# Second MoE of an FFT and two-MoE kernel: seven Strassen products in place of eight block products

## What is computed

```python
def reference(x, moe_w_in, moe_w_out, moe2_w_in, moe2_w_out, moe2_alpha):
    X = np.fft.fft(np.fft.fft(x, axis=1), axis=2).real     # x: 2 x 3008 x 256
    X = X.reshape(6016, 256)
    h = X @ moe_w_in                                        # 256 x 2048
    X1 = (h / (1 + np.exp(-h))) @ moe_w_out                 # 2048 x 256
    h = X1 @ moe2_w_in
    g = np.maximum(h, 0) + moe2_alpha * np.minimum(h, 0)
    return g @ moe2_w_out                                   # 6016 x 256
```

## Time and profile before

| | |
|---|---|
| median of 3 runs | 970.4 us (970.27 to 970.58) |
| profiled execution | 971.95 us |
| its span, first to last instruction | 970.1 us |
| PE matmul, busy | 960.3 us, 99%, 4186 matmuls |
| PE weight loads, busy | 785.5 us, 81% |
| DVE, busy | 433.7 us, 45% |
| ACT, busy | 575.3 us, 59% |
| POOL, busy | 495.7 us, 51% |
| granted TensorE clock | 1.0 (2.4 GHz) throughout |

### The profile page before, as it was taken

One profiled execution on the slowest core, in us unless ns is written; L12 is line 12 of the kernel. 1 busy time (PEld: TensorE's weight loads), 2 busy tenths in 40 slices (PEclk: granted clock), 3 DMA queues, 4 the chain that ended last, 5 costly groups with the idle time before them and its releaser, 6 DMA issues.

```text
span 970.1 us, 10736 instructions
## 1 busy us (share of the span) xinstructions
PE 960.3 (99%) x4186; PEld 785.5 (81%) x4186; DVE 433.7 (45%) x627; ACT 575.3 (59%) x681; POOL 495.7 (51%) x240
## 2 busy tenths in 40 slices
PE   9999999999999999999999999999999999999998
PEld 4578887888888888878888888888888888888887
DVE  6779974655544544554443232322223233232321
ACT  2475654676666666667665556555555655655554
POOL 0197553477656555565755444444535354444533
PEclk9999999999999999999999999999999999999999
DMA  9512000011000000000000000000000000000000
GB/s 347 210 55 64 1 1 1 22 33 54 23 1 22 1 1 0 1 1 23 22 22 1 22 0 22 1 22 22 1 21 1 22 1 22 22 1 21 1 22 22
DMA packets 12776, 27.94 MB, mean 29 GB/s; under 512 B 1290, under 2 KB 8500, under 8 KB 11700
## 3 DMA queue, kind: packets, MB, share of 16 engines
q1 hardware_dynamic: 12628, 27.21, 7.9%
q0 software_dynamic: 96, 0.03, 0.0%
HBM read 21.03 MB, written 6.21 MB: 28 GB/s over the span
## 4 chain that ended last, share of the span: by engine, by line
PE 89%; DVE 5%; POOL 2%; ACT 1%; issue 1%; DMA 1%; SPq 0%; ACTq 0%; DVEq 0%; POOLq 0%
PE ps L309 12%; PE ps L311 12%; PE ps L310 12%; PE ps L561 9%; PE ps L566 9%; PE ps L560 9%; PE ps L526 7%; PE ps L522 7%; PE ps L523 7%; POOL gl L1047 2%; PE ps L470 2%; PE ps L422 1%; DVE h_sb L971 1%; PE ps L454 1%; DVE x_tile L793 1%
## 5 line engine op out<-in xcount | busy, mean ns | idle before, releaser
L1047 POOL TENSOR_TENSOR gl<-g_sb,gh 128x1004 fp32r<-128x1004 f32 x192 | 419.6, 2186 | 430.0 <-ACT gh L700 267.7
L1007 DVE SCALAR_TENSOR_TENSOR g_sb<-h_sb,neg_alpha,g_sb 128x502 f32<-128x502 f32 x192 | 160.4, 877 | 349.9 <-ACT g_sb L695 349.9
L700 ACT CAST gh<-g_sb 128x1004 fp32r<-128x1004 f32 x96 | 99.1, 1032 | 137.9 <-DVE g_sb L1007 137.9
L522 PE MATMUL ps<-gh,wo 128*128 128x502 f32 x384 | 148.0, 386 | 1.0 <-DVE x L961 0.8
L561 PE MATMUL ps<-gh,wo 128*128 128x502 f32 x384 | 148.6, 387 | 0.0
L523 PE MATMUL ps<-gh,wo 128*128 128x502 f32 x384 | 148.4, 386 | 0.0
L309 PE MATMUL ps<-xs,wi 128*128 128x502 f32 x384 | 148.0, 385 | 0.0
L310 PE MATMUL ps<-xs,wi 128*128 128x502 f32 x384 | 148.0, 385 | 0.0
L311 PE MATMUL ps<-xs,wi 128*128 128x502 f32 x384 | 148.0, 385 | 0.0
L560 PE MATMUL ps<-gh,wo 128*128 128x502 f32 x384 | 147.3, 384 | 0.0
L971 DVE SCALAR_TENSOR_TENSOR h_sb<-n_all,a,v_sb 128x502 f32<-128x502 f32 x96 | 81.5, 849 | 144.9 <-ACT v_sb L732 144.9
(11 more groups left out here) (88 smaller groups left out, 1137.2 us busy)
## 6 DMA issues: line engine op xcount, KB each, us to landing
x_tile<-x_tiles SPq DMA_DIRECT2D x6, 1024.0 KB, 13.7
out_t<-out_sb SPq DMA_DIRECT2D x11, 502.0 KB, 2.8
stage<-moe_w_out SPq DMA_DIRECT2D x16, 256.0 KB, 2.8
n_parts<-n_rows SPq DMA_DIRECT2D x5, 502.0 KB, 3.8
w_sb<-moe_w_in SPq DMA_DIRECT2D x4, 512.0 KB, 8.6
stage<-moe_w_in SPq DMA_DIRECT2D x8, 256.0 KB, 4.2
t_sb<-t SPq DMA_DIRECT2D x1, 1134.0 KB, 17.8
t_sb<-t SPq DMA_DIRECT2D x3, 376.0 KB, 13.7
```

Source lines behind the costliest of these rows:

```text
L522: pe.matmul(dst, wh, gh[g % 2][:, sg, :], start=f == 0, stop=False)
L1007: ins = dve.scalar_tensor_tensor(out=gs[:, i, :], in0=m[:, i, :], scalar=neg_alpha[:, f:f + 1], in1=gs[:, i, :], op0=ALU.mult, op1=ALU.add)
L1047: pool.tensor_tensor(gl[g % 2][:, :, :], g_sb[g % 2][:, :, :], gh[g % 2][:, :, :].bitcast(F32), ALU.subtract).then_inc(gl_done, 1)
```

## The change

The product h = w_in^T x of the second MoE is taken as a 2 x 2 block product: w_in's inner features in two halves of 1024 (8 blocks of 128 each), its input features in two halves of 128, and the chunk's tokens in two halves of 502. Strassen's scheme makes the four blocks of h from seven products of sums of blocks. So for each of 48 units (6 chunks by 8 blocks, `UNITS`) there are 7 times `three` = 21 matmuls in place of 24, each product in a bank of its own (banks 0 to 3, three of them used twice). DVE forms the four 128x502 tiles of h from PSUM by seven additions (`half_sum`) into h4 in SBUF, the first of them with product 1, which ACT copies out of PSUM before (`copy_p1`). ReLU, PReLU, rounding and low part are then made from h4 in three portions, tile 0, tile 1, and tiles 2 and 3 together; before, ReLU read PSUM. The second product keeps its 24 matmuls per unit, tile by tile, in banks 4 to 7, all four of which are accumulated through a chunk, and its first half lies between products 7 and 2 of the next unit, its second half behind product 4.

The sums of blocks have to be made and split as well. Of w_in: 4 sums (POOL), 7 roundings (ACT) and 7 low parts (POOL), each in two portions of 512 columns, in steps 38 to 48 and 54 to 64 of the first MoE. Of x1: each chunk is stored to DRAM when it is done (SP) and four of its quarters are loaded back, then 4 sums, 7 low parts (POOL) and 7 roundings (ACT) of 502 columns per chunk, for chunk 0 in steps 71 to 89, for the others in units 1 to 6 of the chunk before. The xs operand and its split go. The eight stage splits of wo2 stand two before unit 0 and two each in units 1 to 3. When a chunk's second product is complete, in the lists of unit 8n of the next chunk, ACT copies banks 6 and 7 and DVE banks 4 and 5 into one output buffer, before PE may start the next chunk's sums in them.

The diff, cut to its core:

```diff
+PRODUCTS = {1: ("a11", "b11"), 6: ("s2", "t2"), 5: ("s1", "t1"), 7: ("s3", "t3"),
+            2: ("a12", "b21"), 3: ("s4", "b22"), 4: ("a22", "t4")}
+W_SETS = ["a11", "a12", "a22", "s1", "s3", "s2", "s4"]
+X_ROWS = ["b11", "b21", "b22", "t1", "t3", "t2", "t4"]
+TILES = [(1, 1), (0, 0), (0, 1), (1, 0)]
...
+        W_AT = [W2_AT + 8192 * i for i in range(4)] + [XS_AT, PQ_AT, PQ_AT + 8192]
...
+        W_SUMS = {"s1": ("a21", "a22"), "s3": ("a11", "a21"), "s2": ("s1", "a11"), "s4": ("a12", "s2")}
...
+        X_SUMS = {"t3": ("b22", "t1"), "t1": ("t1", "b11"), "t2": ("b22", "t1"), "t4": ("b21", "t2")}
+        X_HI = ["b11", "t1", "t4", "b21", "b22", "t3", "t2"]
+        X_STEP_SUM, X_STEP_HI, X_STEP_LO = 71, [75, 76, 77, 85, 86, 87, 88], [76, 77, 78, 86, 87, 88, 89]
...
+            def store_x1(c):
+                for i in range(2):
+                    sp.wait_ge(x1_done[i], c + 1)
+                sp.dma_start(x1_rows[c].rearrange("p a t -> p a t"),
+                             x1[:, c, :, :, :].rearrange("p s j t -> p (s j) t")).then_inc(x1_out, 16)
+            def load_xr(n):
+                sp.wait_ge(x1_out, 16 * max(n + 1, 4 if n == 0 else 0))
+                for k, x in enumerate(("b11", "b21", "t1", "b22")):
+                    sp.dma_start(xr_raw[n % 2][x][:, :], x1_rows[n, :, k, :]).then_inc(xr_in, 16)
...
+            sp.wait_ge(stage_hi, WO2_ITEM)
+            sp.wait_ge(stage_lo, WO2_ITEM)
+            load_w7(0)
+            store_x1(0)
             sp.wait_ge(t1_lo, len(T1_JOBS))
             sp.wait_ge(t23_lo, len(T23_JOBS))
             store_n(NC1 // 2, NC1)
             sp.wait_ge(n_out, 64)
             load_n(3)
-            for i in range(WI2_ITEM + 4, WO2_ITEM):
+            store_x1(1)
+            load_n(4)
+            store_x1(2)
+            sp.wait_ge(w7_lo, len(W_SETS))
+            load_w7(1)
+            load_n(5)
+            store_x1(3)
+            load_xr(0)
+            sp.wait_ge(w7_lo, 2 * len(W_SETS))
+            for i in range(WO2_ITEM, WO2_ITEM + SLOTS):
                 load_item(i)
-            load_n(4)
-            for i in range(WO2_ITEM, WO2_ITEM + 4):
+            store_x1(4)
+            store_x1(5)
+            sp.wait_ge(mm2, STEPS1)
+            load_xr(1)
+            for i in range(WO2_ITEM + SLOTS, len(items)):
                 load_item(i)
...
+            for n in range(NC1):
+                if 1 <= n < NC1 - 1:
+                    sp.wait_ge(prod_b, 3 * HF * n)
+                    load_xr(n + 1)
...
+            def product(u, p):
+                n, fp = divmod(u, HF)
+                w, x = PRODUCTS[p]
+                bank = {1: 0, 6: 1, 5: 2, 7: 3, 2: 0, 3: 1, 4: 2}[p]
+                wh, wl = (w7[w][:, i, fp * P:(fp + 1) * P] for i in range(2))
+                xh, xl = (xr[n % 2][x, i][:, :] for i in range(2))
+                return three(pe, ps[:, bank, 0:N], wh, wl, xh, xl, True, True)
+            def products_a(u):
+                n, fp = divmod(u, HF)
+                if u == 0:
+                    pe.wait_ge(h_done, STEPS1)
+                    pe.wait_ge(w7_lo, 2 * len(W_SETS))
                 if fp == 0:
...
+                    pe.wait_ge(xr_lo, len(X_ROWS) * (n + 1))
+                for i, p in enumerate((1, 6, 5, 7)):
+                    if u and i < 3:
+                        pe.wait_ge(comb, 7 * u - 2 + i)
+                    product(u, p).then_inc(prod_a, 1)
+            def products_b(u):
+                pe.wait_ge(p1_done, u + 1)
+                product(u, 2).then_inc(prod_b, 1)
+                pe.wait_ge(comb, 7 * u + 1)
+                product(u, 3).then_inc(prod_b, 1)
+                pe.wait_ge(comb, 7 * u + 2)
+                product(u, 4).then_inc(prod_b, 1)
+            def second2(u, k):
+                n, fp = divmod(u, HF)
+                half, sg = TILES[k]
+                f = fp + HF * half
                 if n == 0:
...
+                    pe.wait_ge(stage_lo, WO2_ITEM + 1 + WO2_ORDER.index(f // 2))
+                if fp == 0 and k < 2:
+                    pe.wait_ge(x1_done[sg] if n == 0 else out_done[sg], NC1 if n == 0 else n)
+                pe.wait_ge(gh_done, STEPS1 + 3 * u + min(k, 2) + 1)
+                out = [ps[:, 4 + 2 * sg + ft, 0:N] for ft in range(2)]
                 for ft in range(2):
...
+                    wh, wl = (wo2[:, f, i, ft * P:(ft + 1) * P] for i in range(2))
+                    pe.matmul(out[ft], wh, gh4[:, k, :], start=fp == 0 and k < 2, stop=False)
+                    pe.matmul(out[ft], wl, gh4[:, k, :], start=False, stop=False)
+                pe.wait_ge(gl_done, STEPS1 + 3 * u + min(k, 2) + 1)
+                for ft in range(2):
+                    ins = pe.matmul(out[ft], wo2[:, f, 0, ft * P:(ft + 1) * P], gl4[:, k, :],
+                                    start=False, stop=fp == HF - 1 and k >= 2)
...
+            for g in range(LAG, STEPS1):
+                first1(g)
+                second1(g - LAG)
                 if g in JOB_AFTER:
                     job(JOB_AFTER[g])
+            second1(STEPS1 - 2)
+            products_a(0)
+            second1(STEPS1 - 1)
+            products_b(0)
+            for u in range(1, UNITS):
+                products_a(u)
+                second2(u - 1, 0)
+                second2(u - 1, 1)
+                products_b(u)
+                second2(u - 1, 2)
+                second2(u - 1, 3)
+            for k in range(4):
+                second2(UNITS - 1, k)
...
+            def copy_p1(u):
+                act.wait_ge(prod_a, 4 * u + 1)
+                if u:
+                    act.wait_ge(comb, 7 * u - 2)
+                act.copy(p1_sb[:, :], ps[:, 0, 0:N]).then_inc(p1_done, 1)
+            def relu(u, k):
+                act.wait_ge(comb, 7 * u + (3, 5, 7)[k])
+                act.wait_ge(gl_done, STEPS1 + max(3 * (u - 1) + k + 1, 0))
+                ks = slice(k, k + 1 if k < 2 else 4)
+                act.activation(g4[:, ks, :], h4[:, ks, :], ACT.Relu)
+                act.activation(h4[:, ks, :], h4[:, ks, :], ACT.Relu, scale=-1.0).then_inc(relu_done, 1)
+            def split_g_hi(u, k):
+                act.wait_ge(g_done, 3 * u + k + 1)
+                act.wait_ge(mm2, STEPS1 + max(4 * (u - 1) + (k + 1 if k < 2 else 4), 0))
+                ks = slice(k, k + 1 if k < 2 else 4)
+                act.copy(gh4[:, ks, :], g4[:, ks, :]).then_inc(gh_done, 1)
...
+            split_hi(WO2_ITEM + 1)
+            for u in range(UNITS):
+                n, fp = divmod(u, HF)
+                copy_p1(u)
+                if u:
+                    split_g_hi(u - 1, 2)
+                if u == 0:
                     store_x1_minus(NC1 - 1)
-                if fp == LAG - 1 and n >= 1:
+                relu(u, 0)
+                if 1 <= u <= 3:
+                    split_hi(WO2_ITEM + 2 * u)
+                    split_hi(WO2_ITEM + 2 * u + 1)
+                split_g_hi(u, 0)
+                if n + 1 < NC1 and 2 <= fp <= 5:
+                    xr_round(n + 1, 2 * (fp - 2))
+                relu(u, 1)
+                if n + 1 < NC1 and 2 <= fp <= 4:
+                    xr_round(n + 1, 2 * (fp - 2) + 1)
+                relu(u, 2)
+                split_g_hi(u, 1)
+                if fp == 0 and n:
                     store_out(n - 1)
...
+            split_g_hi(UNITS - 1, 2)
+            store_out(NC1 - 1)
+            act.wait_ge(mm2, half_last(NC1 - 1))
+            act.wait_ge(out_dma[0], 16 * (NC1 - 1))
+            act.copy(out_sb[:, 0, 0, :], ps[:, 4, 0:N]).then_inc(last_out[0], 1)
...
+            def half_sum(u, i):
+                bank, dst, other = [(1, 3, None), (2, 2, 3), (3, 0, 2), (3, 3, 3), (0, 1, None), (1, 2, 2), (2, 3, 3)][i]
+                if i < 4:
+                    dve.wait_ge(prod_a, 4 * u + min(2 + i, 4))
+                else:
+                    dve.wait_ge(prod_b, 3 * u + i - 3)
+                if i == 0:
+                    dve.wait_ge(p1_done, u + 1)
+                    dve.wait_ge(g_done, 3 * u)
+                elif i != 4:
+                    dve.wait_ge(comb, 7 * u + (None, 1, 2, 2, None, 3, 4)[i])
+                add = p1_sb[:, :] if other is None else h4[:, other, :]
+                dve.tensor_tensor(h4[:, dst, :], ps[:, bank, 0:N], add, ALU.add).then_inc(comb, 1)
+            def prelu(u, k):
+                dve.wait_ge(relu_done, 3 * u + k + 1)
+                for i in range(k, k + 1 if k < 2 else 4):
+                    f = u % HF + HF * TILES[i][0]
+                    ins = dve.scalar_tensor_tensor(out=g4[:, i, :], in0=h4[:, i, :], scalar=neg_alpha[:, f:f + 1],
+                                                   in1=g4[:, i, :], op0=ALU.mult, op1=ALU.add)
+                ins.then_inc(g_done, 1)
+            def store_out(n):
+                dve.wait_ge(mm2, half_last(n))
+                if n:
+                    dve.wait_ge(out_dma[0], 16 * n)
+                else:
+                    dve.wait_ge(x1_out, 16 * NC1)
```

(72 more changed lines are left out.)

290 lines of the change are left out of this document (125 added, 165 removed).

## The result

The changed kernel takes **984.62 us** (median of 4 runs, 983.39 to 985.24) where the kernel before takes 970.49 beside it: ratio 1.0142, 95% interval 1.0125 to 1.016. The profiled execution took 984.17 us with a span of 982.3; PE's granted clock has a mean of 0.995. The matmuls went as planned (4042 are left of 4186), and 14 us more than their 32 came back as waiting.

What follows compares the result with a forecast made beforehand. PE, busy 99% of the span, was taken as the bound. Gains of 32.2 us against 32.3 paid gave 972.05, less 1.55 to the runs' median and 0.7 for uncounted slack: 969.8 us, no change, range 950 to 980.

Steps and rivals of the forecast that it cites:

- Removed: Second MoE: 144 matmuls go over 48 units at 0.2233 us each, a gross gain of 32.2 us.
- The lock: In each unit's last two PReLUs, POOL's 1.08 us operation goes in between over a shared port, adding 0.87 us.
- the ring: Loop through DVE and ACT from half sum 0 of one unit to the next: 10.11 us against PE's 10.05.
- The faster rival: POOL's request comes behind the second PReLU, the pair runs unbroken, about 19 us saved: 951 us; chance 0.2.
- The ring's sum: Half sums, ReLUs and PReLUs of one unit: 2.13, 1.16, 0.66, 1.88, 2.00 and 1.41, together 9.24 us, without POOL's delay.
- Plain units 0.6: Units without side work: 0.07 us each where the ring leads, two or three in each of four chunks: 0.6 us.
- Edges 10.6: Five chunk edges: PE waits for ACT's and DVE's copies of the result, 2.1 us each, 10.6 us paid.
- x rows 7.6: Next chunk's x rows, ACT copies in the ring in units 2 to 5: 1.9 us in each of four chunks, 7.6.
- First chunk 8.8: 1.6 us for a wait in unit 1 plus 7.2 for stage splits and x rows in units 1 to 6: 8.8.
- End 4.2: Behind the last half sum, PE waits 1.3, 0.3, 1.2 and 1.35 us for the closing operations: 4.2 us paid.
- The slower rival: POOL's new x-row work also blocks other PReLUs, two more hits a chunk: 12 us more, 982 us; chance 0.2.
- The signs: If right: PReLU pairs 2.2 to 2.3 us, plain units 10.05 to 10.15; wrong if POOL's 502-column mean exceeds 1.3 through waiting.

Runs made afterwards that it cites:

- experiment 1: Changed kernel plus one wait: POOL makes tile 1's low part only after DVE's last pair of PReLUs; 966.15 us, ratio 0.9956.
- 7: Changed kernel with POOL's added wait, one wait per dependent half sum, moved x roundings and exchanged edge copies together; 951.66 us, ratio 0.981.
- Experiment 2: Changed kernel with half sum 0 waiting for all first four products and the next three only for the preceding half sum; 976.63 us, ratio 1.0062.
- experiment 3: Changed kernel without making or loading x rows for chunks 1 to 5, whose products read chunk 0's rows; 965.02 us, ratio 0.9943.
- experiment 5: Changed kernel with the edge's copies exchanged: DVE copies banks 6 and 7 before the PReLU pair, ACT the other two; 978.4 us, ratio 1.0085.
- experiment 4: Changed kernel with ACT's x-row roundings moved before the unit's first ReLU, same work; 972.77 us, ratio 1.0023.

## Why the prediction was wrong

**Removed: right.** 144 matmuls at 0.2233 us. In the last chunk of experiments 1 and 7, where nothing else leads, a unit takes 10.05 us as worked out.

**The lock: right, with its size.** Forecast: POOL goes into the seam and puts 0.87 us into the ring. Measured: 0.82 (2.21 against 1.39), 0.54 us after the pair's start. The faster rival, in which POOL loses the race, did not come about by itself; experiment 1 made it happen, and it was worth 18.5 us where its 951 had said about 19. That the two are so near is partly luck: the 19 were counted from a ring that led PE by 0.06, the 18.5 from one that led by 0.30, in a kernel whose x-row units stayed at 11.05. The prediction drew on the Trainium skill, "SBUF — State Buffer", section "SBUF: two separate sides": the one that starts first has the port for the whole instruction. All plain units bear it out, with pairs of 2.21 us. Between two DVE operations that follow each other directly, it was POOL that got it here each time.

**The ring's sum: the step that failed.** "Sum 9.24 us" and with the seam "10.11 us against PE's 10.05" should have been 10.35. Term by term, predicted and measured: sums 0 to ReLU 0, 2.13 and 2.28 (933.69 less 930.24 less ACT's 1.17); ReLUs 1.16 and 1.17; PReLU 0 0.66 and 0.66; sums 4 to 6 1.88 and 1.88; ReLUs of 1004 2.00 and 2.01; the pair to the next half sum 2.28 and 2.34. The six measured terms sum to 10.34. Two terms were too small, both for the same thing, the hand-over from one DVE operation to the next that needs it: the three dependent sums (2.28, not 2.13) and the pair to the next half sum (2.34, not 2.28). I took 0.03 from the earlier trace rows, where the operation waits for its predecessor alone. In the kernel the sums wait for the predecessor and for a product, and there it is 0.10; half sum 0 waits for three things, 0.13 behind the pair. Experiment 2 took the second wait from sums 1 to 3 and the spacing was 0.71 at once. For the 0.13 no run was made, so that it comes from the number of waits is only argued. 0.24 us a unit is nothing by itself, but times 47 it is 11 of the 14.8 us by which the forecast missed (what was wrong at the edges and in the x rows nearly cancels), and it stands in the one term of the sum that has no slack. The sentence "a unit with nothing else in it is a draw" was a draw to 0.06 us between two numbers each good to about 0.1; a range of 963 to 975 for "no change" was too tight for that.

**Plain units 0.6: wrong**, 14.1, for the same reason.

**Edges 10.6: wrong in kind.** The forecast counted PE's waits for the two copies, 2.1 each. PE does wait there, 1.9 us on the weight load for ACT's copy and 0.8 for DVE's. But once the ring leads, PE is early all the time, and a wait at one place takes the place of another. What an edge really costs is what it puts into the ring: 0.89. That the price was 5.4 us too high hid half of the other mistake.

**x rows 7.6: right in place, low in size.** Two copies 0.51 each were put into the ring, "ring 10.1 + 0.51 + 0.27 = 10.9". Measured 10.35 + 0.80 = 11.15, the 0.80 as priced; the one copy of unit 5 0.29 as priced (0.27). What was missed: the 0.7 us of slack granted to each chunk was not there (2.8 us), and the two late transfers cost 1.2 (0.94 and 0.26). "DMA 0" for the x rows was wrong by these: a transfer need not be late for its reader to be late for the lock.

**First chunk 8.8: near** (7.4), though by another route. The splits alone cost nothing (experiment 3) and the x rows alone 0.80; what costs is both together. POOL then has two splits and two x-row operations on top of its own work and comes to the low part of tiles 2 and 3 so late that it lies across PReLU 0 of the next unit, which is why unit 4, with no split of its own, takes 11.98 as well. POOL and DVE in unit 2:

```profile
475.55 2.17 POOL L1276 TENSOR_TENSOR gl<-g,gh 128x1004 fp32r<-128x1004 f32 x1
```

```profile
476.81 1.46 DVE L1156 SCALAR_TENSOR_TENSOR g<-h,neg_alpha,g 128x502 f32<-128x502 f32 x1 [0.62 <-ACT h L823]
```

PReLU 0 takes 1.46 us instead of 0.74 there and about as long in units 3 and 4; the pair of unit 1 takes 3.25 us for the same lateness of POOL, which makes the 12.91. (The 9.0 us of L822 behind POOL's gl in the groups above are another thing: four waits of 2.24 us behind the edges, where POOL's operation and the half sum ended together, and the ReLU started 2.27 us after half sum 0 as everywhere.)

**End 4.2: right in sum, wrong in make-up.** 22.99 us against 22.8. PE waited 1.55, 0.88 and 0.17 us, 2.6 together, and the rest is the clock, below. With the clock at 1.00 (experiment 5) the same end took 21.94 us with 3.5 of waits, so the clock, which no term held, cost 1.05 and made up for waits that were priced too high. **Start 0:** 0.85, not seen; the first L815 lies anywhere from 448.09 to 449.71 in kernels that are the same up to there. **First MoE 0, DMA 0.5:** PE's waits for gl between 180 and 446 us sum to 1.1 us on weight loads, no more than forecast.

**The slower rival** named 982 us, 2.6 from the result, but not by its mechanism: experiment 4 leaves POOL's x-row work as it is and takes away all of its regular cost; only the two units of chunks 1 and 4 were of that kind, 1.2 us, and in the first chunk the three units with PReLU 0 held up, 0.72 each, in place of 12. A number that comes out right by the wrong cause is a miss too.

**The signs.** Pairs of 2.2 us and half sums of 0.67 came as said; plain units at 10.05 to 10.15 did not. Of the signs of being wrong one came: POOL's mean for 502 columns in the second MoE was 1.33 us (1.22 for low parts, 1.51 for x rows) where the prediction had drawn the line at 1.3, and experiment 4 shows that this was nearly free in chunks 1 to 4.

## What to carry to other kernels

When two loops are within a few per cent of each other, the question is which leads, and every hand-over in the slower one is to be priced by an operation with the same number of waits. If a ring leads, count only what lies inside it: waits of the fast engine are where the lost time shows, not what it costs. Then look for the idle stretches of the ring's own engines and move each side job (a copy, a rounding, a store) into one of them, and hold back a helper that would take a shared port in a seam; here four such edits of a few lines turned 1.4% slower into 1.9% faster.
